# Gated delta recurrence on one core: the nine head steps of the block solver moved ahead of the mask of h, and one signal of that mask made two

## The reference, cut to what matters

```python
for t in range(S):
    y[:, :, t] = np.einsum('bhd,bhde->bhe', rt, state)
    Sa = np.einsum('bhde,bhe->bhd', state, at)
    state_decay = state * wt[:, :, None, :] - np.einsum('bhd,bhe->bhde', Sa, bt)
    state = state_decay + np.einsum('bhd,bhe->bhde', vt, kt)
```

## Time and profile before

| | us |
|---|---|
| median of 3 runs | 925.05 (922.23 to 927.7) |
| the profiled execution, its own time | 923.58 |
| its span in the trace | 921.9 |
| PE busy | 824.6 |
| DVE busy | 559.7 |
| ACT busy | 317.4 |
| POOL busy | 259.5 |
| mean granted TensorE clock, share of full speed | 0.946 |

### The profile page before, as it was taken

One profiled execution on the slowest core, in us unless ns is written; L12 is line 12 of the kernel. 1 busy time (PEld: TensorE's weight loads), 2 busy tenths in 40 slices (PEclk: granted clock), 3 DMA queues, 4 the chain that ended last, 5 costly groups with the idle time before them and its releaser, 6 DMA issues.

```text
span 921.9 us, 27713 instructions
## 1 busy us (share of the span) xinstructions
PE 824.6 (89%) x11872; PEld 597.0 (65%) x11872; DVE 559.7 (61%) x1235; ACT 317.4 (34%) x741; POOL 259.5 (28%) x525
## 2 busy tenths in 40 slices
PE   3428989998999988889998999988999998999988
PEld 3428889988998988864465654545644656545555
DVE  8995795878599742136528645357464277354474
ACT  4102331323133232222227542246432266322364
POOL 2087777778778877000000000000000000000000
PEclk9999895979599798899999999999999979999999
DMA  3645575657566574620100000100001000000000
GB/s 117 153 85 122 126 163 113 134 139 140 122 157 138 113 158 102 157 78 26 44 1 15 16 15 1 43 0 23 15 8 43 1 8 22 16 1 0 1 15 30
DMA packets 130922, 61.33 MB, mean 67 GB/s; under 512 B 106544, under 2 KB 119792, under 8 KB 130800
## 3 DMA queue, kind: packets, MB, share of 16 engines
q1 hardware_dynamic: 96156, 32.61, 16.3%
q10 hardware_dynamic: 34644, 26.95, 11.3%
HBM read 45.37 MB, written 14.16 MB: 65 GB/s over the span
## 4 chain that ended last, share of the span: by engine, by line
PE 75%; DVE 11%; issue 5%; ACT 5%; POOL 2%; DMA 1%; SPq 0%; ACTq 0%; DVEq 0%
PE ps_all L808 8%; PE ps_all L792 8%; PE ps_scan L105 5%; PE ps_all L852 5%; PE ps_scan L188 4%; PE ps_all L918 4%; PE ps_all L900 4%; PE ps_all L930 4%; PE ps_scan L130 3%; PE ps_scan L167 3%; PE ps_all L795 3%; PE ps_all L802 2%; PE ps_all L835 2%; PE ps_scan L122 2%; PE ps_scan L114 2%
## 5 line engine op out<-in xcount | busy, mean ns | idle before, releaser
L328 POOL TENSOR_TENSOR t_update<-solver_then_w_down 128x133 f32<-128x133 f32 (+13 forms) x251 | 118.6, 473 | 88.1 <-DMA solver_then_w_down<-l_blocks 39.1
L330 POOL TENSOR_TENSOR solver_then_w_down<-solver_then_w_down,t_update 128x133 f32<-128x133 f32 (+13 forms) x251 | 132.7, 529 | 19.7
L105 PE MATMUL ps_scan<-decayed_a_and_eye,scaled_then_x 40*128 40x104 f32 x768 | 67.6, 345 | 46.5 <-DVE decayed_a_and_eye L362 45.2
L1129 DVE TENSOR_REDUCE minus_max<-ps_all 128x1 f32<-128x128 f32 (+5 forms) x96 | 55.3, 617 | 66.8 <-PE ps_all L904 66.8
L105 PEld LDWEIGHTS ps_scan<-decayed_a_and_eye,scaled_then_x 40*128 40x128 f32 x768 | 62.8, 252 | 48.6 <-issue 47.7
L808 PE MATMUL ps_all<-gated,solver_then_w_down 128*128 128x384 f32 x256 | 91.1, 499 | 0.0
L792 PE MATMUL ps_all<-scaled_then_x,inputs_then_w_up 128*128 128x384 f32 x256 | 88.8, 490 | 1.8 <-ACT ak_l_then_ffn L970 1.8
L1028 ACT ACTIVATE probs_t<-ps_all 128x512 f32<-128x512 f32 (+3 forms) x128 | 55.1, 452 | 69.9 <-PE ps_all L918 69.3
L808 PEld LDWEIGHTS ps_all<-gated,solver_then_w_down 128*128 128x128 f32 x256 | 46.0, 189 | 44.6 <-issue 19.1
L792 PEld LDWEIGHTS ps_all<-scaled_then_x,inputs_then_w_up 128*128 128x128 f32 x256 | 47.6, 190 | 36.3 <-ACT ak_l_then_ffn L970 6.0
L232 ACT ACTIVATE x_rhs<-ps_scan 128x320 f32<-128x320 f32 x48 | 21.0, 438 | 141.3 <-PE ps_scan L122 70.5
(11 more groups left out here) (117 smaller groups left out, 1523.8 us busy)
## 6 DMA issues: line engine op xcount, KB each, us to landing
r_t_and_v_t<-in_rv ACTq DMA_DIRECT2D x48, 160.0 KB
inputs_then_w_up<-in_x ACTq DMA_DIRECT2D x46, 160.0 KB
solver_then_w_down<-l_blocks SPq DMA_DIRECT2D x22, 256.0 KB, 4.6
uv_and_ruv<-in_v ACTq DMA_DIRECT2D x48, 80.0 KB, 3.7
y_t<-y_out SPq DMA_DIRECT2D x24, 160.0 KB
out<-out_rows SPq DMA_DIRECT2D x24, 160.0 KB, 1.8
inputs_then_w_up<-in_x ACTq DMA_DIRECT2D x46, 81.4 KB
inputs_then_w_up<-in_x ACTq DMA_DIRECT2D x46, 80.0 KB
```

The lines of the kernel that those rows point to most:

```text
L105: last = nc.tensor.matmul(PS[:, o:o + ROWS], weights, AL[c % NK][rows(h), p, :], start=True, stop=True)
L328: return (lambda: eng.tensor_tensor(tmp[:, 0:cols, 0:rest], l[:, s:s + 1, s + 1:BLK].broadcast_to(shape), t[:, 0:cols, s:s + 1].broadcast_ ...
L330: lambda: eng.tensor_tensor(t[:, 0:cols, s + 1:BLK], t[:, 0:cols, s + 1:BLK], tmp[:, 0:cols, 0:rest], ALU.subtract))
L1129: nc.vector.tensor_reduce(NM[:, v:v + 1], PS[:, first_bank(v) * 512:first_bank(v) * 512 + n], AX.X, ALU.min).then_inc(m["nm"], 1)
```

## The change

The constant FIRST goes, and `solve_head` does all nine steps of a pair in one piece ahead of the mask of h. Each of the two instructions of that mask now increments `hm`, so its count is twice what it was: the squares wait for the first half (2n - 1) at their start and for the second (2n) before the four products of the other two banks, and `gain_and_out` waits for 2(n + 1).

```diff
         def g_products(c, n):
             if n >= 1:
-                pe.wait_ge(m["hm"], n)
+                pe.wait_ge(m["hm"], 2 * n - 1)
...
             for p in range(P8):
+                if n >= 1 and p == 4:
+                    pe.wait_ge(m["hm"], 2 * n)
                 for h in range(2):
                     o = place(2 * h, p)
...
         def gain_and_out(n):
             if n + GA >= NT:
-                pe.wait_ge(m["hm"], n + 1)
+                pe.wait_ge(m["hm"], 2 * (n + 1))
...
         def hm(n):
             dve.wait_ge(m["h"], n + 1)
             for h in range(2):
-                i = nc.vector.tensor_tensor(UV[n % 3][:, h, :, D:ROWS], by8(PH[h], C),
-                                            MK[:, :].unsqueeze(1).broadcast_to([128, P8, C]), ALU.mult)
-            i.then_inc(m["hm"], 1)
+                nc.vector.tensor_tensor(UV[n % 3][:, h, :, D:ROWS], by8(PH[h], C),
+                                        MK[:, :].unsqueeze(1).broadcast_to([128, P8, C]), ALU.mult).then_inc(m["hm"], 1)
...
-        def solve_head(j, steps, last):
-            if steps.start == 0:
-                dve.wait_ge(m["l_in"], 32 * j)
...
+        def solve_head(j):
+            dve.wait_ge(m["l_in"], 32 * j)
...
-            for s in steps:
+            for s in range(HEAD):
                 mult, sub = step(nc.vector, LU[j % 2], TS[j % 2], TMD, s)
                 link(dve, mult())
-                if s < last:
+                if s < HEAD - 1:
                     link(dve, sub())
                 else:
                     sub().then_inc(m["head"], 1)
...
             if n % 2 == 1 and 2 <= pair < NPAIR:
-                first = HEAD if pair == 2 else FIRST
-                solve_head(pair, range(0, first), HEAD - 1)
+                solve_head(pair)
                 hm(n - 1)
-                solve_head(pair, range(first, HEAD), HEAD - 1)
```

More of the change, by code:

```diff
@@ L28 @@
 PAD = 118
-FIRST = 4
 PARTS = {"w": slice(0, WCOLS + 1), "a": slice(WCOLS + 1, WCOLS + 1 + HC), "kb": slice(WCOLS + 1 + HC, XCOLS)}
@@ L393, in y_out @@
                                     two(pf3(n)[:, :, 0:C]), ALU.mult).then_inc(m["yo"], 1)
-        def solve_head(j, steps, last):
-            if steps.start == 0:
-                dve.wait_ge(m["l_in"], 32 * j)
[L398 to L402, removed]
-            for s in steps:
+        def solve_head(j):
+            dve.wait_ge(m["l_in"], 32 * j)
+            dve.wait_ge(m["eye"], j + 1)
+            if j == 2:
+                dve.wait_ge(m["solved_first"], 1)
+            else:
+                dve.wait_ge(m["head"], j - 2)
+            for s in range(HEAD):
                 mult, sub = step(nc.vector, LU[j % 2], TS[j % 2], TMD, s)
                 link(dve, mult())
-                if s < last:
+                if s < HEAD - 1:
                     link(dve, sub())
```

## The result

| | before | after |
|---|---|---|
| median of 22 runs each, us | 922.51 | 924.35 |
| ratio | | 1.0069, 95% interval 1.0040 to 1.0098 |
| profiled execution, own time | 923.58 | 929.18 |
| its span, mean granted clock | 921.9, 0.946 | 927.4, 0.948 |

What follows compares the result with a forecast made beforehand. PE, 89% busy, was taken to set the pace. Mask waits of 4.80 us less 0.86 and 1.16 at n=19 and 20 gave +2.8; stalls cut this to +1.5, 926.5 us on 925.05. Range 921.5 to 931.2.

Steps and rivals of the forecast that it cites:

- The squares wait for the mask, 4.80 in all: Squares on PE start late in odd iterations because head steps precede the mask of h: 4.80 us added up to n=17.
- Where: Squares wait 0.81, 0.52, 0.81, 1.12, 1.54 us at n=7, 9, 13, 15, 17; none at n=3, 5, 11.
- Same steps, 2.86: On VectorE, steps 4 to 8 keep their duration when moved ahead of the mask: 2.86 us at n=7 and 9.
- Two signals save 0.60 per wait, 3.0 in all: The mask's first half opens PE 0.60 us sooner than one end signal, at five waits; the second wait never bites.
- The solver starts sooner: GpSimd's solver starts 1.21 us sooner at n=7, 9, 13, 15, 17 and 3 to 5 at n=3, 5, 11.
- Stalls without a releaser pay for the waits: PE stalls of unknown cause absorb added mask waits; only n=7 counted, 0.8 of 2.8 us, plus about half a us.
- Rival B: Tail at n=17 to 24 shifts too, nothing taken back: 6.6 us slower, 931.7 us; chance 0.09.
- C: PE's stalls absorb the added waits wholly and the last solver parts start 1.21 us sooner: 923.8 us; chance 0.15.
- Rival D: Idle time on PE brings one more low-clock stretch, at most 4.5 us, 6.0 with the forecast: 931.1 us; chance 0.09.
- E: The solver's loop bounds more than waits show; its 1.21 us passes on five times: -6.0, 919.0 us; chance 0.07.
- F: h comes late in all odd iterations, head steps fill idle time, the change does nothing: 925.0 us; chance 0.08.

Runs made afterwards that it cites:

- the second set: The changed kernel run once more without any edit, beside the kernel before on one chip: median 919.2 us, ratio 1.0025 to the kernel before.
- late weights: SyncE issues the next stage's weights at n=22 instead of n=18: in the kernel before 919.23 us (0.9984), in the changed kernel 921.22 us (1.0004).
- the added delay: Changed kernel with six memsets on VectorE between the head's end and the mask of h, n=3 to 19: 955.98 us, ratio 1.0355 to the kernel before.
- order alone: Kernel before with all nine head steps ahead of the mask but one signal at its end: 928.95 us (1.0108), again 926.47 us (1.0070).
- Mask first: Kernel before with all nine head steps moved behind the mask of h, one signal: 930.01 us, ratio 1.0085 to the kernel before.

## Why the prediction was right or wrong

The forecast was +1.5 us, 926.5 on the median of 925.05, and "within 0.5%" with a chance of 0.75. The median of 924.35 lies in the range and the medians moved by +1.84, but the ratio of 1.0069 lies above 0.5%, and its interval reaches from 0.4% to 1.0%. So the sign was right and so was the mechanism, that the late mask holds the squares. That 1.84 comes so near to 1.5 is in part luck: the standard error of the difference is 1.7, and the terms below came out otherwise one by one. The range of 921.5 to 931.2 says little by itself, since it also holds the 922.51 of the kernel before; its centre came from three runs whose median, 925.05, was 2.5 above that of 22. By the times at equal clock (2 to 4) the forecast took back too much.

- **The squares wait for the mask, 4.80 in all.** About right: 4.2 in the profile shown, 6.8 in that of the second set, 6.5 in the one with late weights. That it passes on to everything behind it was shown by the added delay.
- **Where.** Partly wrong. Waits were forecast at n = 7, 9, 13, 15 and 17 and none at 3, 5 and 11. In the profile shown they are at 3, 9 and 15, in that of the second set at every odd n from 5 to 17, with late weights at 7, 9, 13 and 17. In the profile shown the squares of n = 17 started without waiting, because PE was slow there (a granted clock of 0.73 in 309 to 313). So whether an iteration waits changes from execution to execution. The granted clock of its stretch is a likely reason, since the squares take 2.04 or 3.74 with it while the mask takes 1.29 at either level; I had read the cover of n = 3, 5 and 11 from one execution as if it belonged to the iteration.
- **"Same steps, 2.86".** This term was mis-sized for some iterations. In the earlier trace rows steps 4 to 8 ran while the solver stood idle waiting for them, as in five of the nine odd iterations before. Ahead of the mask they start sooner and the solver is more often still at the pair before. At n = 9 the head took 6.5 instead of about 5.2, and the wait was 1.74 where 0.52 was forecast: the 1.2 between them is about the lengthening. Over all nine iterations the five steps took 2.4 us more, 29.5 against 27.1. The row of n = 15, 3.60, had said so, and I used it for that iteration alone. The Trainium skill has this rule (SBUF — State Buffer, "Who interferes with whom"): a VectorE `tensor_tensor` with both inputs in SBUF contends with GpSimd's reads. The trace agrees: 0.41 against 0.23 for the same shape, and steps 4 to 8 took 2.86 to 2.89 wherever the solver was idle, and up to 3.9 where it worked beside them.
- **Two signals save 0.60 per wait, 3.0 in all.** The 0.60 is right: 0.73 from the start of the mask to the squares against 1.33 with one signal. The sum is not shown: order alone waited 6.8 and 9.5 in its two profiles, the change 4.2 to 6.8. In time at equal clock the gain is between -0.3 and 1.5; not settled further. In the old order they give nothing, as forecast.
- **The solver starts sooner.** In this pair of profiles right in direction: its wait for the head fell by 9.3, about the 10 named. Between executions it varies as much: over 90 to 400 us it was 27.6, 23.8 and 20.4 in three profiles of the old order, and 17.4, 23.9 and 10.5 in three of the changed kernel. What I did not count is that a sooner solver may pay PE outside n = 19 and 20. In the same three profiles of the old order PE waited 2.0, 4.0 and 5.6 for x_rhs behind the inverse blocks, in the three of the changed kernel not at all, nor in the two of order alone. That is a likely reason why waits of 4 to 7 cost only 2 to 4; against it, the old order with eight head steps shows no such wait either, and no experiment took it apart.
- **Stalls without a releaser pay for the waits.** Not borne out, and it is what moved the forecast from 2.8 to 1.5. Ahead of x_from_state they were 5.4 before, 8.9, 6.0 and 7.6 in the changed kernel, and 7.0 with the delay. Ahead of all products together, over 90 to 400 us, they were 18.3 before and 18.7 after; between executions they ran from 8.4 to 18.3 in the old order, so a payment of 1.3 could not be seen. By the times at equal clock +2.8 is the better sum, by the medians +1.5. The rule of the Trainium skill weighed in the prediction (Runtime: NRT & Kernel Launch, "Instruction fetch mechanics") says that fetching instructions is mostly hidden; no run here shows what these stalls are.
- **Rival B** (6.6, nothing taken back). Not seen at its size: 931.7 against 924.35. Its sign, the stretch from n = 17 to the end of the recurrence longer by over 5, is there in the pair of profiles (97.5 against 86.8), but the same stretch took 87 to 102 in four profiles of the old order, so it decides nothing. Its thought that the wait passes on in full was right. **C** (sooner by the solver) falls, since no set of the changed kernel is sooner than the kernel before at equal clock.
- **Rival D** (clock). The change itself ran at 0.952 and 0.956 against 0.952 to 0.954 for the kernel before, so no extra stretch on the whole. But single waits were followed by one. PE was busy 2.28 of the 4 us of 280 to 284, with the wait of n = 15 in them, and from 284 to 292 the clock was 0.50 and the squares took 3.74. Around the wait of n = 9 it was busy 2.26 of 4, and the clock was 0.70 from 200 to 204. The kernel before had such stretches without these waits, and no run shows that the waits brought them. Mask first and order alone had 0.942, 0.943 and 0.950. Such shifts are worth more than the change: 0.01 of clock is 6 us by the fit, and the times at equal clock leave this out. **E and F** fall: the squares wait, and nothing became faster.

## What to carry to other kernels

Before a block is moved ahead of a signal on an engine that has little slack, ask who stands behind it in its old and in its new place, and whether its inputs are there; here the head costs the squares in one place, the state in another, and in a third it waits for its own blocks and holds up the transposes. Take a duration from a row only together with what ran beside it: steps that are short because their partner waits for them can become longer when that wait is removed. And where the clock moves the time by more than the change does, compare runs at equal clock and enlarge the suspected cost until it stands out.

## What was not expected of the hardware

Between executions of one and the same kernel the mean granted clock ran from 0.939 to 0.964 (22 runs of the changed kernel), and the times from 932.48 to 916.48 with it. Kernels that do the same work with other waits had means from 0.942 (mask first) to 0.956, and the one with the delay 0.939. Mask first and the delay lie further below the kernel before on their chips (0.952 and 0.954) than their runs' scatter explains: by 0.009 and 0.015, with standard errors of 0.003 and 0.004. What sets this was not tried.

A multiply of 128x81 on VectorE took 0.23 us with GpSimd idle and 0.41 beside its solver, and the head of nine steps, up to the start of the mask, 4.7 us with the solver idle throughout (order alone, n = 7) and up to 6.6 beside a busy one (late weights in the changed kernel, n = 7).
